# The last 128 tokens of the last product: tokens held in the array instead of the weights, their result stored a token a row, their other half stored ahead

## The reference

```python
x = attention_in_chunks(q, k, v)                 # (4608, 512)
xn = x / sqrt(mean(x * x) + 1e-6) * rms_g
x = (silu(xn @ w_gate) * (xn @ w_val)) @ w_out   # first net
h = x @ w_in                                     # second net
g = h * clip(h + 3.0, 0.0, 6.0) / 6.0
out = g @ w_out2                                 # (4608, 512), float32
```

## Time and profile before

| | |
|---|---|
| median of 3 runs | 1644.12 us (1643.08 to 1645.68) |
| the profiled execution | 1643.31 us, span of its core 1641.5 us |
| PE busy | 1602.5 us (98%) |
| DVE, ACT, POOL busy | 64%, 52%, 49% |
| granted TensorE clock | 0.995 of full speed |
| DMA | 366.88 MB, mean 223 GB/s |

### The profile page before, as it was taken

One profiled execution on the slowest core, in us unless ns is written; L12 is line 12 of the kernel. 1 busy time (PEld: TensorE's weight loads), 2 busy tenths in 40 slices (PEclk: granted clock), 3 DMA queues, 4 the chain that ended last, 5 costly groups with the idle time before them and its releaser, 6 DMA issues.

```text
span 1641.5 us, 29728 instructions
## 1 busy us (share of the span) xinstructions
PE 1602.5 (98%) x11332; PEld 1569.7 (96%) x11332; DVE 1048.4 (64%) x1436; ACT 859.0 (52%) x1341; POOL 797.8 (49%) x779
## 2 busy tenths in 40 slices
PE   6899999999999999999999999999999999999998
PEld 5698999999999999999999999999999999999998
DVE  5778878867755445755455776665666865455454
ACT  5576766755544444644444565554665654434432
POOL 2753443558866664523230377687675631231231
PEclk9899999999999999999999999999999999999999
DMA  9686876635565655989997856647648986676674
GB/s 175 151 197 152 200 192 168 174 117 173 166 231 189 210 193 204 370 313 313 311 312 281 297 206 232 239 173 254 217 175 299 373 265 200 218 228 212 212 229 118
DMA packets 335646, 366.88 MB, mean 223 GB/s; under 512 B 186256, under 2 KB 299152, under 8 KB 332304
## 3 DMA queue, kind: packets, MB, share of 16 engines
q1 hardware_dynamic: 319472, 334.16, 64.4%
q0 software_dynamic: 8800, 28.85, 5.2%
q10 hardware_dynamic: 7232, 1.97, 0.7%
HBM read 200.80 MB, written 164.10 MB: 222 GB/s over the span
## 4 chain that ended last, share of the span: by engine, by line
PE 85%; DMA 3%; DVE 3%; issue 3%; ACT 3%; POOL 2%; SPq 1%; ACTq 0%; DVEq 0%; POOLq 0%
PE bx L993 14%; PE by L993 14%; PE bx L994 13%; PE bx L995 13%; PE by L994 13%; PE by L995 13%; DMA hl_b<-h_scratch 1%; PE att L962 1%; DVE tx L1531 1%; PE att L918 1%; PE att L971 1%; PE att L941 1%; ACT tx L1179 1%; DMA v_first<-in_v_dram 1%; DMA h_scratch<-ht 1%
## 5 line engine op out<-in xcount | busy, mean ns | idle before, releaser
L993 PE MATMUL bx<-tx,wr 128*128 128x384 f32 x840 | 285.5, 340 | 6.5 <-DVE tx L1531 4.2
L993 PE MATMUL by<-tx,wr 128*128 128x384 f32 x840 | 285.8, 340 | 2.2 <-DVE vb L1557 1.5
L995 PE MATMUL bx<-tx,wr 128*128 128x384 f32 x840 | 281.3, 335 | 0.0
L994 PE MATMUL by<-tx,wr 128*128 128x384 f32 x840 | 281.3, 335 | 0.0
L995 PE MATMUL by<-tx,wr 128*128 128x384 f32 x840 | 281.2, 335 | 0.0
L994 PE MATMUL bx<-tx,wr 128*128 128x384 f32 x840 | 281.2, 335 | 0.0
L1583 DVE TENSOR_TENSOR hl_d<-hl_d 128x1536 fp32r<-128x1536 f32 x84 | 147.2, 1786 | 93.7 <-ACT hl_d L1280 93.5
L1903 POOL DMA_DIRECT2D out_dram<-ot x128 | 70.2, 556 | 248.8 <-DVE ot L1606 246.3
L1583 DVE TENSOR_TENSOR hl_b<-hl_b 128x1152 fp32r<-128x1152 f32 x84 | 119.1, 1433 | 107.2 <-ACT hl_b L1280 106.8
L1280 ACT ACTIVATE hl_d<-hl_d 128x1536 fp32r<-128x1536 f32 x84 | 123.1, 1485 | 114.6 <-DMA hl_d<-u_scratch 114.6
L993 PEld LDWEIGHTS bx<-tx,wr 128*128 128x128 f32 x840 | 158.2, 188 | 10.9 <-DVE tx L1531 5.7
(11 more groups left out here) (205 smaller groups left out, 3783.0 us busy)
## 6 DMA issues: line engine op xcount, KB each, us to landing
hl_d<-u_scratch SPq DMA_DIRECT2D x84, 768.0 KB, 4.4
hl_b<-h_scratch SPq DMA_DIRECT2D x84, 576.0 KB, 5.9
u_scratch<-ut SPq DMA_DIRECT2D x48, 576.0 KB, 3.7
h_scratch<-ht SPq DMA_DIRECT2D x36, 576.0 KB, 3.8
u_scratch<-ub SPq DMA_DIRECT2D x96, 192.0 KB, 3.1
u_scratch<-ub SPq DMA_DIRECT2D x48, 384.0 KB, 2.5
h_scratch<-vb SPq DMA_DIRECT2D x72, 192.0 KB, 3.2
h_scratch<-vb SPq DMA_DIRECT2D x36, 384.0 KB, 3.6
```

What stands on the lines that cost most here:

```text
L993: pe.matmul(dst, w_hi, m_hi, start=start, stop=False, skip_group_check=not opens)
L994: pe.matmul(dst, w_hi, m_lo, start=False, stop=False, skip_group_check=not opens)
L995: return pe.matmul(dst, w_lo, m_hi, start=False, stop=stop, skip_group_check=not opens)
```

## The change

The 128 columns of the last run are done with the operands' roles swapped. For each `kt` the tokens' block of `hl_d` (128 x 128) is loaded into the array, and the 256 weight columns of both streams stream through it, again three passes; the result in `att` has tokens in partitions and 256 features in columns. So that what is already there can be added, PE first turns `o_last` (two 128 x 128 transposes against `ident` into another bank of `att`), and DVE copies that to a new tile `o_by_token`. Behind the product DVE adds both once, into `o_last`, ordered as the rows of the output. SP stores the first 64 tokens (partitions 0 to 63), ACT the other 64, each with one DMA in pieces of 64 features (256 bytes). The block `O11` of these tokens is stored ahead in pieces of 256 bytes too: four DMAs by SP and four by ACT, as soon as it is turned; behind them come the stores of the 256 columns as before.

```diff
-        for r, run in enumerate(LAST_RUNS):
-            sp.wait_ge(last_turned, 2 * r + 2)
-            for g, hf in LAST_SHARES[0]:
-                src, dst = rows_out(NSB - 1, 0, run, g, hf)
-                sp.dma_start(dst, src).then_inc(last_stored_sp, 16)
-        sp.wait_ge(last_stored_sp, 16 * 8)
-        sp.wait_ge(last_stored_act, 16 * 8)
+        for g, hf in LAST_SHARES[0]:
+            src, dst = rows_first_half(g, hf)
+            sp.dma_start(dst, src).then_inc(last_stored_sp, 16)
+        sp.wait_ge(last_turned, 2)
+        for g, hf in LAST_SHARES[0]:
+            src, dst = rows_out(NSB - 1, 0, LAST_RUNS[0], g, hf)
+            sp.dma_start(dst, src).then_inc(last_stored_sp, 16)
+        sp.wait_ge(last_added, 1)
+        src, dst = rows_last_half(0)
+        sp.dma_start(dst, src).then_inc(last_stored_sp, 16)
+        sp.wait_ge(last_stored_sp, 16 * 9)
+        sp.wait_ge(last_stored_act, 16 * 9)
...
+                for st in range(2):
+                    tr = pe.transpose(att[:, 1, st * P:(st + 1) * P], o_last[:, st], ident[:, :])
+                tr.then_inc(last_by_token, 1)
+                for kt in range(kn):
+                    hl = half_buf(ph, half_of(s, o, kt // (kn // 2)))[:, :, kt % (kn // 2), LAST_COLS[1]]
+                    dst = att[:, 0, 0:2 * P]
+                    pe.matmul(dst, hl[:, HI], w[:, HI, kt], start=kt == 0, stop=False)
+                    pe.matmul(dst, hl[:, LO], w[:, HI, kt], start=False, stop=False)
+                    mm = pe.matmul(dst, hl[:, HI], w[:, LO, kt], start=False, stop=kt == kn - 1)
+                mm.then_inc(last_prod, 1)
...
+        def add_last():
+
+            dve.wait_ge(last_by_token, 1)
+            dve.tensor_copy(o_by_token[:, :], att[:, 1, 0:2 * P]).then_inc(last_sum_copied, 1)
+            dve.wait_ge(last_prod, 3)
+            dve.wait_ge(last_sum_copied, 1)
+            whole = o_last[:, :, :].rearrange("p h (g2 t n) -> p t (h g2) n", g2=2, t=2)
+            dve.tensor_tensor(whole, att[:, 0, 0:2 * P].rearrange("p (t g n) -> p t g n", t=2, g=4),
+                              o_by_token[:, :].rearrange("p (t g n) -> p t g n", t=2, g=4), ALU.add).then_inc(last_added, 1)
```

More of the change, by code:

```diff
@@ L137, in chunked_attention_then_two_ffns @@
     o_last = at("o_last", [P, 2, P], F32, U0 + 95232)
+    o_by_token = at("o_by_token", [P, 2 * P], F32, U0 + 36864)
     CONST = U0 + 97216
@@ L270, in chunked_attention_then_two_ffns @@
     last_copied = sem("last_copied")
+    last_by_token = sem("last_by_token")
+    last_sum_copied = sem("last_sum_copied")
     last_added = sem("last_added")
@@ L1041, in down_product @@
                     accumulator_free(m, o, st)
[L1042 to L1049, removed]
+                for st in range(2):
+                    for kt in range(kn):
+                        hl = half_buf(ph, half_of(s, o, kt // (kn // 2)))[:, :, kt % (kn // 2), LAST_COLS[0]]
+                        mm = three_passes(bank(m, st, ROLE[o])[:, LAST_COLS[0]], weight(HI, kt, st), weight(LO, kt, st),
+                                          hl[:, HI], hl[:, LO], False, kt == kn - 1, False)
+                    mm.then_inc(last_prod, 1)
+                for st in range(2):
+                    tr = pe.transpose(att[:, 1, st * P:(st + 1) * P], o_last[:, st], ident[:, :])
+                tr.then_inc(last_by_token, 1)
+                for kt in range(kn):
+                    hl = half_buf(ph, half_of(s, o, kt // (kn // 2)))[:, :, kt % (kn // 2), LAST_COLS[1]]
[3 more added lines that the diff above has]
+                    mm = pe.matmul(dst, hl[:, HI], w[:, LO, kt], start=False, stop=kt == kn - 1)
+                mm.then_inc(last_prod, 1)
         def keep_busy(times, there=by[:, 0, :]):
@@ L1316, in relu, with store_last @@
             act.activation(relu_to(i), src, ACT.Relu, bias=half[:, 0:1], scale=1.0 / 6.0).then_inc(relu_done, 1)
-        def store_last(run):
+        def store_last():
+            act.wait_ge(turned, turned_no(NSB - 1, O11, 1))
             for g, hf in LAST_SHARES[1]:
-                src, dst = rows_out(NSB - 1, 0, run, g, hf)
+                src, dst = rows_first_half(g, hf)
                 act.dma_start(dst, src).then_inc(last_stored_act, 16)
+            act.wait_ge(last_turned, 2)
+            for g, hf in LAST_SHARES[1]:
+                src, dst = rows_out(NSB - 1, 0, LAST_RUNS[0], g, hf)
+                act.dma_start(dst, src).then_inc(last_stored_act, 16)
+            act.wait_ge(last_added, 1)
+            src, dst = rows_last_half(1)
+            act.dma_start(dst, src).then_inc(last_stored_act, 16)
         for n in range(4):
@@ L1467, in _ @@
                 splits(m, o)
[L1468 to L1472, removed]
+        store_last()
+        act.wait_ge(last_stored_act, 16 * 9)
     @block.vector
@@ L1606, in turn, with turn_last @@
             dve.transpose(turned_of(s, i, st), src.rearrange("p (b t) -> p b t", t=TB)).then_inc(turned, 1)
[L1608 to L1616, removed]
+        def turn_last(st):
+            dve.wait_ge(last_prod, st + 1)
+            src = bank(D0 + NSB - 1, st, "a")[:, LAST_COLS[0]]
+            dve.transpose(turned_of(NSB - 1, O21, st, LAST_COLS[0]), src.rearrange("p (b t) -> p b t", t=TB)).then_inc(last_turned, 1)
+        def add_last():
[6 more added lines that the diff above has]
+                              o_by_token[:, :].rearrange("p (t g n) -> p t g n", t=2, g=4), ALU.add).then_inc(last_added, 1)
         def comb_c(m, which, st):
@@ L1777, in _ @@
                 splits(m, o)
-        for cols in LAST_COLS:
-            for st in range(2):
-                turn_last(st, cols)
+        for st in range(2):
+            turn_last(st)
+        add_last()
     @block.gpsimd
```

## The result

| | before | changed kernel |
|---|---|---|
| median, 22 runs each | 1643.24 us (1637.84 to 1646.80) | 1638.86 us (1633.89 to 1647.65) |
| the profiled execution | 1643.31 us, span 1641.5 | 1641.36 us, span 1639.6 |
| ratio | | 0.9976, 95% interval 0.9966 to 0.9986 |

Faster, by 0.24%, or 2.3 to 5.6 us.

What follows compares the result with a forecast made beforehand. PE alone, then an uncovered tail of DVE and stores, bounds the end; PE -2.23, DVE -0.21, issues -1.37 and landing +0.4 sum to -3.4 us, from 1644.12 to 1640.7 us, range 1639.3 to 1643.0.

Steps and rivals of the forecast that it cites:

- What bounds the end: From 1631.70 us PE alone sets the time, then a 4.2 us tail of DVE and stores that nothing covers.
- PE: Last product: 24 matmuls at 0.119 us replace 48 at 0.110, two transposes cost 0.22 us; -2.23 us, bounds -2.3 and -2.0.
- Rival 2: Last product: swapped matmuls take 0.22 us each and gain nothing on PE; sum -1.1 us, 1643.0 us; chance 0.05.
- DVE and issues: Tail: one 0.42 us add saves 0.21 us, the copy is hidden, one store issue per queue saves 1.37 us.
- Landing: Last store, from issue to arrival: 2.1 us against 1.7 before, so +0.4 us, bounds -0.1 and +1.1.
- between them, for 256 pieces, 1.0 us: Last store's wait for its first packet, put between 0.83 us (64 or 128 pieces) and 1.4 us (512-piece load).
- The level and its allowance: Whole kernel: starting median 1644.12 us, and about 1 us added on either side for medians of few runs.
- The border of 0.2%: Whole kernel: 1640.8 us divides faster from same; chances: faster 0.45, same 0.51, slower 0.04.
- The rule against it: Final stores: skill's read-modify-write below 512 bytes could make 256-byte pieces slow, giving -2.3 us instead of -3.4.
- rival 1: Final stores: a 256-byte piece costs twice a 512-byte one; landing 3.2 us, sum -2.3 us, 1641.8 us; chance 0.20.
- Rival 3: DMA engines behind SP's and ACT's queues: last stores choke at 0.24 us a piece; +3.6 us, 1647.7 us; chance 0.03.

Runs made afterwards that it cites:

- the later comparison: The changed kernel run once more, unaltered, beside the kernel before: 1638.97 us (12 runs) against 1642.13 us (35 runs), ratio 0.9978.

## Why the prediction was wrong

**What bounds the end: right.** PE alone, then a tail that nothing covers; all of it came off the span.

**PE: right, to the hundredth.** -2.23 us, at the steps priced from the earlier trace rows and the transposes of the earlier trace rows. The first product starts 0.14 us behind the first transpose, the second one 0.20 us later, and the other 22 steps, from 1633.30 to 1635.93, are 0.1195 us each: 0.14 for the transposes and 0.08 lost behind them make the 0.22 us of the forecast. Rival 2 (0.22 us a matmul) is refuted by the timeline.

**DVE and issues: right.** 0.42 us for the add, the copy under cover, and one issue for each queue at the forecast place.

**Landing: mis-sized.** The step "between them, for 256 pieces, 1.0 us" to the first packet failed. The rows it was drawn from differed in pieces, 64, 128 and 512, but the extra time doesn't go by pieces: 64 pieces took 1.15 us in one form and 0.8 in another. It was 1.2 us, data took 0.8 instead of 0.6, and the landing of ACT's store 2.4 us instead of 2.1, within the bounds of 1.6 and 2.8. (The 1638.8 at which the prediction ends before's wait for the first packet stands in none of the rows that it names; the trace has the packet at 1638.80.) That made the end 3.05 to 3.14 us shorter, not 3.4.

**The level and its allowance: the step that put the time outside the range.** The prediction took 1644.12 us, the median of three runs, as the level, and "about 1 us on either side" for medians of few runs, of which 0.7 us went below its own bound of 1640.0. In the comparison itself before's median over 22 runs is 1643.24 us: the level was 0.9 us too high. That alone would have stayed within the range, for 1643.24 - 3.05 is 1640.2. The changed kernel's median lies another 1.3 us lower, at 1638.86, and the end piece doesn't show these 1.3 us. The interval of the ratio, 2.3 to 5.6 us, holds 3.05, and the later comparison gave 3.2; so they may be no more than the spread of medians, but something ahead of the end isn't excluded, and the cause stays open. Later medians of before, in part on other chips, were lower still: 1642.13 (35 runs), 1642.73 (9) and 1641.59 (17). The two misses of the level and its spread, 2.2 us, outweigh the landing, which missed by 0.35 us the other way. The border of 0.2%, on which the chances were split, isn't decided: the ratio says 0.24%, the end pieces say 3.1/1642 = 0.19%, and the intervals hold both.

**The rule against it.** The page "DMA: Bandwidth & Descriptors" of the Trainium skill (Specifications) has a read-modify-write below 512 bytes. The run with only the stores changed shows no cost of it here: landing 1.5 us on SP's queue and 1.6 on ACT's with 256 bytes, 1.6 and 1.7 with 512. So rival 1, for which the rule was cited, is refuted at this load. Rival 3, the choking of the queue, falls too: it wanted a landing above 5 us, and the changed kernel's took 2.4.

## What to carry to other kernels

Where 128 or fewer columns stream through weights of 128 x 128, the matmul is paced by something that is fixed, here 0.11 us at the full clock; swap the roles so that 256 stream, and half of the matmuls go. In a tail that nothing covers, stores issued one behind another cost 0.45 us each, and everything that doesn't depend on the last product can be stored ahead. When single runs spread over 9 us and the effect is 3, compare the piece that the change touches, from an event common to both traces, and take the level from many runs before giving a range around it.

## What the runs showed of the hardware

The end piece is the same within 0.1 us in both pairs of like executions (9.81 and 9.81 us, 6.76 and 6.67 us); what varies is what lies ahead of it. The last `by` matmul of 14 profiled kernels, on PE the same work up to there, starts between 1624.42 and 1636.43 us. It goes in part with the granted clock of the first 140 us: six with 0.95 start between 1628.67 and 1636.43, five with 0.98 between 1624.42 and 1630.60. Here are before, the slowest and the fastest (columns: stretch, us, busy of PE, PEld, DVE, ACT, POOL, granted clock, DMA share, GB/s):

```profile
0.00:140.00 140.00, 115.92 (x1518) 98.81 (x1519) 103.25 (x167) 85.47 (x153) 76.20 (x83) 0.95 0.82 172
```

```profile
0.00:140.00 140.00, 115.98 (x1512) 97.99 (x1515) 102.89 (x166) 84.96 (x153) 75.48 (x83) 0.95 0.84 172
```

```profile
0.00:140.00 140.00, 119.24 (x1573) 100.95 (x1574) 105.97 (x175) 88.75 (x158) 75.22 (x83) 0.98 0.83 174
```

Three hundredths of 140 us are 4 us of the array at full clock, by estimate. The rest of the 12 us wasn't traced. Part of it may go by chip: on one the four starts lie between 1630.73 and 1636.43, on a second between 1626.10 and 1630.60, on a third (three starts) between 1627.00 and 1628.67. The medians of before on these three differ by only 1.1 us.

I hadn't expected that a store's form moves its issue from 0.43 to 0.65 us and its first packet from 0.8 to 1.3 us, with the same bytes and the same number of pieces; nor that a stretch with half the columns would come out longer, by way of the clock.
